# An attention stage and two gated MLPs in split float32 on one core: the norm's sum over partitions as two split products, output tiles stored one by one, and a third weight piece prepared earlier

## The chip, the cores and the metric

The kernel runs on one core of a Trainium2 chip. The metric is the device time of one execution in microseconds. The engines of the core are called PE (TensorE), DVE (VectorE), ACT (ScalarE), POOL (GpSimd) and SP (SyncE, which here only issues transfers).

## What is computed

The reference takes q, k and v of shape (4, 8, 576, 64). For each head it adds two attentions: one over tokens averaged in groups of four, and one over the neighbours closer than four positions. The result, seen as 2304 tokens by 512 features, goes through two MLPs:

```python
h = x @ w_in                                   # 512 -> 2048
x = (max(h, 0) + alpha * min(h, 0)) @ w_out    # 2048 -> 512

xn = x / sqrt(mean(x * x, axis=-1) + 1e-6) * rms_g
g, val = xn @ w_gate, xn @ w_val               # 512 -> 1536, twice
out = (g * sigmoid(g) * val) @ w_out2          # 1536 -> 512
```

## The kernel before

**Split products.** The large products keep float32 accuracy with operands of the type float32r. An operand is written as hi, its rounded copy (made by ACT with a Copy), and lo, the rest (operand minus hi, made by DVE, or by POOL for part of the weights). A product is then three: hi with hi, hi with lo and lo with hi, all summed in one PSUM bank. The weights come in pieces of 128x512; `piece_hi` on ACT and `piece_lo` on DVE or POOL split them. Pieces 0, 2 and 4 (`EARLY`) get their lo from DVE; pieces 6, 8 and 10 (`EARLY_POOL`) are split by POOL alone. The piece 2c is the w_in part that chunk c of the first MLP needs.

**Opening.** The first half batch of attention is computed alone, in an order written out by hand for each engine: `FIRST_PE`, `FIRST_ACT` and `FIRST_DVE`. A letter is a step and the number after it is a head pair: A loads and transposes q and k, B makes scores, P, E and F are the softmax, C transposes the probabilities, D makes the attention's result in `xbuf`. X splits one quarter of the token block (`xhi` by ACT, then `xlo` by DVE), H splits off a weight piece's hi on ACT, L its lo on DVE, and W on PE is work that only keeps the engine busy. Every engine runs its own list in order and waits on semaphores for the others. An H or an X on ACT must precede the L or the X of the same number on DVE; X also needs D of that number done by DVE.

**First MLP.** It goes over 8 blocks of 288 tokens (`TB1`), each in 16 chunks (`C1`) of 128 hidden features. Chunk c: `up` (12 products of 288 columns), then ACT and DVE make the leaky ReLU and its split (`pos`, `neg`, `g1hi`, `g1lo`), and `down` for the chunk two back (12 products). The steps of the next half batch's attention are placed between chunks. In the first block, `up` of chunk 1 waits for the lo of piece 2.

**Second MLP.** It goes over 6 blocks of 384 tokens (`TB2`), each in 12 chunks (`C2`): `up2` is 24 products of 384 columns, `down2` of the chunk two back is 9 products of 512 columns, three for each output tile `y_b[0]`, `y_b[1]`, `y_b[2]` of 128 tokens. The next block's norm is made meanwhile: ACT squares the block (`sq`), DVE sums the four quarters (`ss`, 128x384), PE sums over partitions with a product of a matrix of ones and `ss`, both plain float32, into `ms_b`; ACT takes the root (`norm_root`), and DVE the reciprocal and the scaling (`norm_scale`). The constants say after which chunk ACT and DVE square and sum, when PE multiplies, and when the root and scaling stand in the queues: `NORM1` in the last block of the first MLP (for block 0), `NORM2` in the second MLP:

```python
    NORM1, NORM2 = (5, 10, 10), (6, 7, 7)
```

**Output.** After a block's last `down2`, ACT copies tiles 0 and 2 and DVE copies tile 1 from PSUM to `ysb`. Both wait for `s_g2_used`, which PE raises once after the last product of `down2`; SP stores the tiles in the order 0, 1, 2.

Of the kernel before, what the change touches and what calls it, by code (L numbers as in the profile page):

```python
# [5 lines left out]
def attention_into_two_mlps_kernel(nc: bass.Bass, q, k, v, w_in, w_leaky, alpha, w_gate, w_val, w_out, rms_g, out):  # L6
# [7 lines left out]
    f32, f32r = mybir.dt.float32, mybir.dt.float32r  # L14
# [65 lines left out]
    FIRST_PE = "W8 A0 W2 A1 W2 B0 W2 A2 W3 B1 A3 W6 B2 K0 W1 C0 W1 B3 W4 D0 W8 C1 W3 C2 D1 W1 C3 D2 D3"  # L80
    FIRST_ACT = "A0 A1 A2 P0 E0 A3 P1 E1 C0 H0 P2 E2 D0 P3 E3 C1 X0 K0 C2 D1 C3 D2 X1 D3 X2 X3 H2 H4"
    FIRST_DVE = "A0 A1 B0 A2 B1 F0 A3 B2 B3 F1 D0 F2 F3 X0 D1 L0 D2 X1 D3 X2 X3 L2 L4"

# [16 lines left out]

    NORM1, NORM2 = (5, 10, 10), (6, 7, 7)

# [6 lines left out]
    with ctx:  # L109
# [9 lines left out]
        eps_out = sb("eps_out", [P, 1])  # L119
        ones = sb("ones", [P, P])  # L120
        loaded = ExitStack()
        W_raw = sb("W_raw", [P, Q1, 2, PIECE], f32, loaded)
# [52 lines left out]
        sq = sb("sq", [P, KT * TB2], f32, part2)  # L175
        ss = sb("ss", [P, TB2], f32, part2)
        rinv = sb("rinv", [P, TB2], f32, part2)
        xnhi = sb("xnhi", [P, KT, TB2], f32r, part2)
# [67 lines left out]
        s_sq = sem("s_sq")  # L246
        s_ss = sem("s_ss")
        s_ms = sem("s_ms")
        s_rms = sem("s_rms")
# [8 lines left out]
        s_g2lo = sem("s_g2lo")  # L258
        s_g2_used = sem("s_g2_used")
        s_y_act = sem("s_y_act")  # L260
        s_y_dve = sem("s_y_dve")
# [378 lines left out]
        def _(act):  # L640
# [93 lines left out]
            def norm(i):  # L734
                act.wait_ge(s_x2_in, 16 * i + 16)
                act.activation(sq[:, :], xn[:, :], ACT.Square).then_inc(s_sq, 1)

            def norm_root(i):
                act.wait_ge(s_ms, i + 1)
                act.activation(rinv[:, :], ms_b[:, 0:TB2], ACT.Sqrt, bias=eps6[:, :], scale=1.0 / DM  # L740
                               ).then_inc(s_rms, 1)
# [18 lines left out]
            def y_out(i):  # L760
                act.wait_ge(s_g2_used, C2 * (i + 1) + BEGUN)
                act.wait_ge(s_y_out, 16 * YT * i + BEGUN)
                for t in (0, 2):
                    act.activation(ysb[:, t, :], y_b[t][:, :], ACT.Copy).then_inc(s_y_act, 1)

            def first_mlp(b, half, group, last=False, pieces=False):
                for c in range(C1):
                    run_steps(group, 2 * c)
                    chunk_relu(b, half, c)
                    run_steps(group, 2 * c + 1)  # L770
                    chunk_hi(b, half, c)
                    if pieces:
                        for n in SPLIT_IN_CHUNK[c]:
                            piece_hi(n)
                    if last:
                        for n in LAST_PIECES[c]:
                            piece_hi(n)
                        if c == NORM1[0]:
                            norm(0)
                        if c == NORM1[2]:  # L780
                            norm_root(0)
# [17 lines left out]
            for kind, p, j in first_order(FIRST_ACT):  # L799
# [6 lines left out]
                elif kind in "PE":  # L806
                    first_softmax(kind, p)
                else:
                    attention(0, 0, kind, p, j)
            first_mlp(0, 0, (0, 1), pieces=True)  # L810
            with act.Fori(0, B - 2) as b:
# [6 lines left out]
            def second_mlp(i, more):  # L818
                for c in range(C2):
# [4 lines left out]
                    if more and c == NORM2[0]:  # L824
                        norm(i + 1)
                    if more and c == NORM2[2]:
                        norm_root(i + 1)
# [11 lines left out]
        def _(dve):  # L839
# [123 lines left out]
            def norm(i):  # L963
                dve.wait_ge(s_sq, i + 1)
                dve.tensor_reduce(ss[:, :], sq[:, :].rearrange("p (t s) -> p s t", t=KT), axis=AX.X, op=ALU.add
                                  ).then_inc(s_ss, 1)

            def norm_scale(i):
# [23 lines left out]
            def y_out(i):  # L992
                dve.wait_ge(s_g2_used, C2 * (i + 1) + BEGUN)
                dve.wait_ge(s_y_out, 16 * YT * i + BEGUN)
                dve.tensor_copy(ysb[:, 1, :], y_b[1][:, :]).then_inc(s_y_dve, 1)

            def first_mlp(b, half, group, last=False):
                for c in range(C1):
# [4 lines left out]
                    if last:  # L1003
# [3 lines left out]
                        if c == NORM1[0]:  # L1007
                            norm(0)
                        if c == NORM1[2]:
                            norm_scale(0)  # L1010
# [29 lines left out]
            def second_mlp(i, more):  # L1040
                for c in range(C2):
# [5 lines left out]
                    if more and c == NORM2[0]:  # L1047
                        norm(i + 1)
                    if more and c == NORM2[2]:
                        norm_scale(i + 1)  # L1050
# [11 lines left out]
        def _(pe):  # L1062
# [99 lines left out]
            def norm(i):  # L1162
# [3 lines left out]
                else:  # L1166
                    pe.wait_ge(s_rms, i)
                pe.wait_ge(s_ss, i + 1)
                pe.matmul(ms_b[:, 0:TB2], ones[:, :], ss[:, :], start=True, stop=True).then_inc(s_ms, 1)

            def first_mlp(b, half, group, last=False):
                for c in range(C1):
# [3 lines left out]
                    if c >= LAG1:  # L1176
                        down(b, half, c - LAG1)
                    if last and c == NORM1[1]:
                        norm(0)
# [53 lines left out]
            def down2(i, c):  # L1233
# [7 lines left out]
                for t in range(YT):  # L1241
                    hi, lo = (g[:, c % 3, t * P:(t + 1) * P] for g in (g2hi, g2lo))
                    for j, (g, w) in enumerate(((hi, 0), (hi, 1), (lo, 0))):
                        last = pe.matmul(y_b[t][:, :], g, wpiece(piece, w), start=(c == 0 and j == 0),  # L1244
                                         stop=(c == C2 - 1 and j == 2))
                last.then_inc(s_g2_used, 1)

            def second_mlp(i, more):
                for c in range(C2):
                    up2(i, c)  # L1250
                    if c >= LAG2:
                        down2(i, c - LAG2)
                    if more and c == NORM2[1]:
                        norm(i + 1)
# [33 lines left out]
```

## Time and profile before

| | |
|---|---|
| median of three runs | 1013.38 us (1012.98 to 1015.3) |
| the profiled execution's own time | 1013.07 us |
| its span, first to last instruction | 1011.3 us |
| what lies around the span | 1.8 us |
| mean granted TensorE clock | 0.997 |
| PE busy | 988.5 us, 98% of the span |
| DVE, ACT, POOL busy | 523.4, 403.4, 113.4 us |

A row of the timeline has a start, a duration, the engine, the line, the operation, what it writes and reads, and the count of instructions merged in it; in square brackets stands the idle time of the engine before it and what ended it. Instructions of one engine overlap a little in such rows, so the distance between starts can be shorter than a duration. A matmul's duration contains its way through the array: the distance from one to the next is what a product costs in a stream. The chain of work gives such distances.

### The profile page before, as it was taken

Reading aid. Unit: us, or ns where it says so; the run is one execution under the profiler, and the core shown is the slowest. Engines: PE = TensorE matmul, PEld = TensorE weight load, DVE = VectorE, ACT = ScalarE, POOL = GpSimd, SP = SyncE. Lnnn points to the kernel's source line nnn. Section 1 sums busy time; section 2 is a strip of 40 time slices with the busy share of each in tenths; the row PEclk is TensorE's granted clock in tenths of the full one; section 3 lists DMA queues with packets and bytes.
Section 4 is the critical chain, followed back from the end, with each engine's and each line's share of the span. In section 5 each row is a group of like instructions: output and inputs, shape, how many; then the busy total and the mean of one; then the engine's idle time right before and its main releaser. Section 6 shows DMA issues by size and latency. Waiting matters only on the chain.

```text
span 1011.3 us, 19296 instructions
## 1 busy us (share of the span) xinstructions
PE 988.5 (98%) x7207; PEld 939.7 (93%) x7207; DVE 523.4 (52%) x955; ACT 403.4 (40%) x953; POOL 113.4 (11%) x122
## 2 busy tenths in 40 slices
PE   8889999999999999999999999999999999999998
PEld 7789999998999999999999999999999999999997
DVE  6887875765766757666456453242242242242211
ACT  6656444445444445444455443232232232232211
POOL 3665310002200012000011221000000000000000
PEclk9999999999999999999999999999999999999999
DMA  8931311113201032010154400100100100100000
GB/s 165 267 94 37 95 37 36 33 43 82 51 20 48 11 99 59 20 49 2 52 178 149 121 1 24 40 1 23 40 0 24 38 0 27 36 0 29 4 1 31
DMA packets 98800, 52.19 MB, mean 52 GB/s; under 512 B 60564, under 2 KB 92840, under 8 KB 98728
## 3 DMA queue, kind: packets, MB, share of 16 engines
q1 hardware_dynamic: 94584, 50.14, 17.9%
q10 hardware_dynamic: 4144, 1.03, 0.7%
q8 instruction: 51, 0.84, 0.3%
q14 instruction: 21, 0.17, 0.0%
HBM read 41.72 MB, written 9.44 MB: 51 GB/s over the span
## 4 chain that ended last, share of the span: by engine, by line
PE 90%; DVE 5%; issue 2%; ACT 2%; DMA 1%; SPq 0%; ACTq 0%; DVEq 0%
PE banks L1229 30%; PE banks L1158 19%; PE banks L1144 17%; PE banks L1244 15%; PE banks L1098 2%; PE banks L1125 2%; PE banks L1109 2%; PE banks L1087 1%; DVE pos L945 1%; PE banks L1113 1%; PE banks L1130 1%; PE banks L1101 1%; PE banks L1192 1%; DMA q_tok_first<-in_q_dram 1%; DVE sm L901 0%
## 5 line engine op out<-in xcount | busy, mean ns | idle before, releaser
L1229 PE MATMUL banks<-xnhi,W_front 128*128 128x384 f32 x672 | 175.9, 335 | 0.0
L986 DVE TENSOR_TENSOR g<-banks,silu 128x384 f32<-128x384 f32 x72 | 40.1, 557 | 236.6 <-ACT silu L755 236.6
L1158 PE MATMUL banks<-g1hi,W_front 128*128 128x288 f32 x640 | 145.9, 304 | 0.0
L1144 PE MATMUL banks<-xhi,W_front 128*128 128x288 f32 x640 | 144.5, 302 | 1.2 <-DVE W_front L843 1.0
L755 ACT ACTIVATE silu<-banks 128x384 f32<-128x384 f32 x72 | 35.4, 492 | 259.7 <-PE banks L1229 259.7
L1229 PEld LDWEIGHTS banks<-xnhi,W_front 128*128 128x128 f32 x672 | 121.9, 188 | 1.3
L945 DVE SCALAR_TENSOR_TENSOR pos<-neg,coef,pos 128x288 f32<-128x288 f32 x128 | 76.8, 600 | 81.6 <-ACT neg L718 81.5
L1229 PE MATMUL banks<-xnlo,W_front 128*128 128x384 f32 x336 | 112.4, 335 | 0.0
L1158 PEld LDWEIGHTS banks<-g1hi,W_front 128*128 128x128 f32 x640 | 107.7, 189 | 3.6 <-issue 3.6
L1144 PEld LDWEIGHTS banks<-xhi,W_front 128*128 128x128 f32 x640 | 107.5, 189 | 3.1 <-DVE W_front L843 1.3
L717 ACT ACTIVATE pos<-banks 128x288 f32<-128x288 f32 x128 | 52.2, 408 | 130.5 <-PE banks L1144 130.3
L1229 PE MATMUL banks<-xnhi,W_back 128*128 128x384 f32 x384 | 103.2, 339 | 0.0
L1144 PE MATMUL banks<-xlo,W_front 128*128 128x288 f32 x320 | 94.9, 297 | 0.0
L1158 PE MATMUL banks<-g1lo,W_front 128*128 128x288 f32 x320 | 94.9, 297 | 0.0
L724 ACT ACTIVATE g1hi<-pos 128x288 fp32r<-128x288 f32 x128 | 56.5, 441 | 89.1 <-DVE pos L945 88.7
L952 DVE TENSOR_TENSOR g1lo<-pos,g1hi 128x288 fp32r<-128x288 f32 x128 | 59.0, 461 | 53.5 <-ACT g1hi L724 53.5
L1144 PE MATMUL banks<-xhi,W_back 128*128 128x288 f32 x384 | 84.5, 296 | 0.0
L1158 PE MATMUL banks<-g1hi,W_back 128*128 128x288 f32 x384 | 83.8, 301 | 0.8 <-DVE g1lo L952 0.8
L1229 PEld LDWEIGHTS banks<-xnhi,W_back 128*128 128x128 f32 x384 | 69.7, 188 | 1.5
L1244 PE MATMUL banks<-W_front,g2hi 128*128 128x512 f32 x216 | 67.2, 392 | 0.0
L1158 PEld LDWEIGHTS banks<-g1hi,W_back 128*128 128x128 f32 x384 | 63.3, 188 | 2.3 <-issue 1.2
L1144 PEld LDWEIGHTS banks<-xhi,W_back 128*128 128x128 f32 x384 | 64.2, 188 | 0.1
(151 smaller groups left out, 1894.0 us busy)
## 6 DMA issues: line engine op xcount, KB each, us to landing
W_raw<-in_moe_w_out_dram SPq DMA_DIRECT2D x26, 256.0 KB, 4.8
x_scratch<-xbuf SPq DMA_DIRECT2D x8, 576.0 KB, 3.5
xn<-x_scratch SPq DMA_DIRECT2D x6, 768.0 KB, 4.6
out_dram<-ysb SPq DMA_DIRECT2D x18, 256.0 KB, 2.2
vwin<-in_v_dram SPq DMA_DIRECT2D x90, 51.0 KB
W_raw<-in_moe_w_in_dram SPq DMA_DIRECT2D x16, 256.0 KB, 5.6
q_tok<-in_q_dram SPq DMA_DIRECT2D x56, 72.0 KB, 2.1
v<-in_v_dram SPq DMA_DIRECT2D x26, 144.0 KB
```

Of the source, the lines that this page charges most:

```text
L717: act.activation(pos[:, c % 2, :], hb[c % 2][:, 0:TB1], ACT.Relu).then_inc(s_pos, 1)
L724: act.activation(g1hi[:, c % 3, :], pos[:, c % 2, :], ACT.Copy).then_inc(s_ghi, 1)
L755: act.activation(silu[:, c % 2, :], gate_b[c % 2][:, 0:TB2], ACT.Silu).then_inc(s_silu, 1)
L945: dve.scalar_tensor_tensor(out=pos[:, c % 2, :], in0=neg[:, c % 2, :], scalar=coef[:, c:c + 1], in1=pos[:, c % 2, :], op0=ALU.mult, op1=AL ...
L952: dve.tensor_tensor(g1lo[:, c % 3, :], pos[:, c % 2, :], g1hi[:, c % 3, :].bitcast(f32), ALU.subtract).then_inc(s_glo, 1)
L986: dve.tensor_tensor(g2[:, c % 2, :], val_b[c % 2][:, 0:TB2], silu[:, c % 2, :], ALU.mult).then_inc(s_g2, 1)
L1098: pe.matmul(scores[0:QW, e, w * KW:(w + 1) * KW], qT[rows[e], p % 2, q0:q0 + QW], kT[rows[e], p, k0:k0 + KW], start=True, stop=True)
L1109: pe.transpose(turned[0:KW, e, w * QW:(w + 1) * QW], sm[:, e, w * KW:(w + 1) * KW], ident[0:QW, 0:QW])
L1144: last = pe.matmul(hb[c % 2][:, 0:TB1], w, x[:, t, :], start=(t + j == 0), stop=(t == KT - 1 and j == 2))
L1158: last = pe.matmul(acc[t][:, 0:TB1], w, g[:, c % 3, :], start=(c == 0 and j == 0), stop=(c == C1 - 1 and j == 2))
L1229: last = pe.matmul(bank[:, 0:TB2], w, x[:, t, :], start=(t + j == 0), stop=(t == KT - 1 and j == 2))
L1244: last = pe.matmul(y_b[t][:, :], g, wpiece(piece, w), start=(c == 0 and j == 0), stop=(c == C2 - 1 and j == 2))
```

## The change

Four edits:

1. **Norm.** `ss` is split as other operands are: ACT writes `sshi` (a Copy, 128x384) and DVE writes `sslo` (a subtraction). PE's one float32 product becomes two float32r products, a copy `ones_r` of the ones with `sshi` and with `sslo`, summed in `ms_b`. ACT makes `ones_r` once (128x128), ahead of its first chunk.
2. **Places of the norm.** The constants now mean: square and sum; split; product, root and scaling. `NORM1` is (5, 8, 10): PE's product stays behind chunk 10, the splits come behind chunk 8. `NORM2` is (6, 7, 8): the splits come behind chunk 7, and product, root and scaling move from chunk 7 to chunk 8.
3. **Output tiles.** PE raises a new semaphore `s_y_tile` after the last product of tile 0 and of tile 1. ACT's copy of tile 0 and DVE's copy of tile 1 wait for it; the copy of tile 2 still waits for `s_g2_used`.
4. **Opening.** H2 goes from the end of ACT's list to behind C2. On DVE, L0 goes ahead of D1, L2 from the end to behind D1, and X1 goes ahead of D2.

```diff
-    FIRST_ACT = "A0 A1 A2 P0 E0 A3 P1 E1 C0 H0 P2 E2 D0 P3 E3 C1 X0 K0 C2 D1 C3 D2 X1 D3 X2 X3 H2 H4"
-    FIRST_DVE = "A0 A1 B0 A2 B1 F0 A3 B2 B3 F1 D0 F2 F3 X0 D1 L0 D2 X1 D3 X2 X3 L2 L4"
+    FIRST_ACT = "A0 A1 A2 P0 E0 A3 P1 E1 C0 H0 P2 E2 D0 P3 E3 C1 X0 K0 C2 H2 D1 C3 D2 X1 D3 X2 X3 H4"
+    FIRST_DVE = "A0 A1 B0 A2 B1 F0 A3 B2 B3 F1 D0 F2 F3 X0 L0 D1 L2 X1 D2 D3 X2 X3 L4"
-    NORM1, NORM2 = (5, 10, 10), (6, 7, 7)
+    NORM1, NORM2 = (5, 8, 10), (6, 7, 8)
...
+            def norm_hi(i):
+                act.wait_ge(s_ss, i + 1)
+                if not isinstance(i, int) or i > 0:
+                    act.wait_ge(s_ms, i)
+                act.activation(sshi[:, :], ss[:, :], ACT.Copy).then_inc(s_sshi, 1)
...
             def y_out(i):
-                act.wait_ge(s_g2_used, C2 * (i + 1) + BEGUN)
                 act.wait_ge(s_y_out, 16 * YT * i + BEGUN)
                 for t in (0, 2):
+                    if t == YT - 1:
+                        act.wait_ge(s_g2_used, C2 * (i + 1) + BEGUN)
+                    else:
+                        act.wait_ge(s_y_tile, (YT - 1) * i + t + 1)
                     act.activation(ysb[:, t, :], y_b[t][:, :], ACT.Copy).then_inc(s_y_act, 1)
...
+            act.wait_ge(s_consts, 2 + NW)
+            act.activation(ones_r[:, :], ones[:, :], ACT.Copy).then_inc(s_eps, 1)
             first_mlp(0, 0, (0, 1), pieces=True)
...
+            def norm_lo(i):
+                dve.wait_ge(s_sshi, i + 1)
+                if not isinstance(i, int) or i > 0:
+                    dve.wait_ge(s_ms, i)
+                dve.tensor_tensor(sslo[:, :], ss[:, :], sshi[:, :].bitcast(f32), ALU.subtract).then_inc(s_sslo, 1)
...
             def y_out(i):
-                dve.wait_ge(s_g2_used, C2 * (i + 1) + BEGUN)
+                dve.wait_ge(s_y_tile, (YT - 1) * i + 2)
...
-                pe.wait_ge(s_ss, i + 1)
-                pe.matmul(ms_b[:, 0:TB2], ones[:, :], ss[:, :], start=True, stop=True).then_inc(s_ms, 1)
+                pe.wait_ge(s_eps, 3)
+                pe.wait_ge(s_sslo, i + 1)
+                pe.matmul(ms_b[:, 0:TB2], ones_r[:, :], sshi[:, :], start=True, stop=False)
+                pe.matmul(ms_b[:, 0:TB2], ones_r[:, :], sslo[:, :], start=False, stop=True).then_inc(s_ms, 1)
...
-                    if last and c == NORM1[1]:
+                    if last and c == NORM1[2]:
                         norm(0)
...
+                    if c == C2 - 1 and t < YT - 1:
+                        last.then_inc(s_y_tile, 1)
                 last.then_inc(s_g2_used, 1)
...
-                    if more and c == NORM2[1]:
+                    if more and c == NORM2[2]:
                         norm(i + 1)
```

## Rows read from the trace of the kernel before

**Rows 1.** The page: busy time by engine, and the chain by line.
```profile
PE 988.5 (98%) x7207; PEld 939.7 (93%) x7207; DVE 523.4 (52%) x955; ACT 403.4 (40%) x953; POOL 113.4 (11%) x122
...
PE banks L1229 30%; PE banks L1158 19%; PE banks L1144 17%; PE banks L1244 15%; PE banks L1098 2%; PE banks L1125 2%; PE banks L1109 2%; PE banks L1087 1%; DVE pos L945 1%; PE banks L1113 1%; PE banks L1130 1%; PE banks L1101 1%; PE banks L1192 1%; DMA q_tok_first<-in_q_dram 1%; DVE sm L901 0%
```

**Rows 2.** PE's waits from 34 us on, the largest: total, times, longest.
```profile
PE banks L1109 <- DVE sm L905: 5.0, 5, 1.8
```

**Rows 3.** The chain around a norm product: start, distance, what.
```profile
599.19 0.65 PE banks L1169 x2
599.84 4.17 PE banks L1229 x24
```

**Rows 4.** Timelines of ACT and DVE, one late block of the second MLP.
```profile
901.03 0.53 ACT L758 ACTIVATE g2hi<-g 128x384 fp32r<-128x384 f32 x1 [0.62 <-DVE g L986]
```
```profile
901.59 0.56 DVE L989 TENSOR_TENSOR g2lo<-g,g2hi 128x384 fp32r<-128x384 f32 x1 [0.59 <-ACT g2hi L758]
```

**Rows 5.** Timelines of PE, ACT and DVE in the first MLP's last block.
```profile
541.66 0.37 PE L1158 MATMUL banks<-g1hi,W_back 128*128 128x288 f32 x1 [0.79 <-DVE g1lo L952]
```
```profile
530.71 0.41 ACT L717 ACTIVATE pos<-banks 128x288 f32<-128x288 f32 x1 [0.21 <-PE banks L1144]
...
533.41 1.28 ACT L740 ACT_TABLE_LOAD   x1
```
```profile
530.53 0.69 DVE L843 TENSOR_TENSOR W_front<-W_raw,W_front 128x512 fp32r<-128x512 f32 x1
...
535.32 2.55 DVE L970 RECIPROCAL rinv<-rinv 128x384 f32<-128x384 f32 x1 [1.96 <-ACT rinv L740]
```

**Rows 6.** Timeline of DVE, 30 to 39 us.
```profile
30.75 0.46 DVE L927 TENSOR_TENSOR xbuf<-banks,od 128x288 f32<-128x288 f32 x1
31.12 1.12 DVE L843 TENSOR_TENSOR W_front<-W_raw,W_front 128x512 fp32r<-128x512 f32 x1
32.88 0.46 DVE L927 TENSOR_TENSOR xbuf<-banks,od 128x288 f32<-128x288 f32 x1 [0.63 <-ACT od L701]
...
34.40 2.23 DVE L934 TENSOR_TENSOR xlo<-xbuf,xhi 128x288 fp32r<-128x288 f32 x2
36.56 2.36 DVE L843 TENSOR_TENSOR W_front<-W_raw,W_front 128x512 fp32r<-128x512 f32 x2
```

**Rows 7.** Timelines of POOL, ACT and PE, 30 to 39 us.
```profile
31.10 0.61 POOL L600 CAST W_front<-W_raw 128x512 fp32r<-128x512 f32 x1 [0.35 <-DMA W_raw<-in_moe_w_in_dram]
...
34.25 1.28 POOL L604 TENSOR_TENSOR W_front<-W_raw,W_front 128x512 fp32r<-128x512 f32 x1
...
36.40 1.37 POOL L604 TENSOR_TENSOR W_front<-W_raw,W_front 128x512 fp32r<-128x512 f32 x1
```
```profile
31.71 0.89 ACT L696 ACTIVATE pT<-banks 102x864 f32<-102x864 f32 x1 [0.99 <-PE banks L1113]
```
```profile
34.58 0.44 PE L1087 MATMUL banks<-ident,q_tok 96*128 96x96 f32 x3 [0.92 <-DVE xbuf L927]
...
38.37 0.41 PE L1144 MATMUL banks<-xhi,W_front 128*128 128x288 f32 x1 [1.02 <-DVE W_front L843]
```

**Rows 8.** The end: the chain's last pieces, the stores, SP's wait.
```profile
1000.64 6.18 PE banks L1244 x27
```
```profile
1006.84 1.09 ACT L764 ACTIVATE ysb<-banks 128x512 f32<-128x512 f32 x2 [4.52 <-PE banks L1244]
...
1007.47 1.31 SPq L479 DMA_DIRECT2D out_dram<-ysb  x3
```
```profile
DMA to landing us min/median/max: 2.0/2.4/2.5
```

**Rows 9.** Windows: us, busy PE, PEld, DVE, ACT, POOL, granted clock, DMA share, GB/s.
```profile
67.00:69.00 2.00, 0.48 (x4) 0.24 (x2) 2.00 (x5) 1.19 (x3) 0.15 (x1) 1.00 0.00 0
70.50:75.00 4.50, 4.50 (x26) 4.48 (x25) 3.02 (x5) 3.42 (x7) 3.11 (x3) 0.62 0.15 36
1008.30:1010.40 2.10, 0.00 (x0) 0.00 (x0) 0.00 (x0) 0.00 (x0) 0.00 (x0) 0.79 0.96 373
```

More of the change, by code:

```diff
@@ L120, in attention_into_two_mlps_kernel @@
         ones = sb("ones", [P, P])
+        ones_r = sb("ones_r", [P, P], f32r)
         loaded = ExitStack()
@@ L176, in attention_into_two_mlps_kernel @@
         ss = sb("ss", [P, TB2], f32, part2)
+        sshi = sb("sshi", [P, TB2], f32r, part2)
+        sslo = sb("sslo", [P, TB2], f32r, part2)
         rinv = sb("rinv", [P, TB2], f32, part2)
@@ L247, in attention_into_two_mlps_kernel @@
         s_ss = sem("s_ss")
+        s_sshi = sem("s_sshi")
+        s_sslo = sem("s_sslo")
         s_ms = sem("s_ms")
@@ L259, in attention_into_two_mlps_kernel @@
         s_g2_used = sem("s_g2_used")
+        s_y_tile = sem("s_y_tile")
         s_y_act = sem("s_y_act")
@@ L779, in first_mlp @@
                             norm(0)
+                        if c == NORM1[1]:
+                            norm_hi(0)
                         if c == NORM1[2]:
@@ L825, in second_mlp @@
                         norm(i + 1)
+                    if more and c == NORM2[1]:
+                        norm_hi(i + 1)
                     if more and c == NORM2[2]:
@@ L964, in norm @@
                 dve.wait_ge(s_sq, i + 1)
+                if not isinstance(i, int) or i > 0:
+                    dve.wait_ge(s_sslo, i)
                 dve.tensor_reduce(ss[:, :], sq[:, :].rearrange("p (t s) -> p s t", t=KT), axis=AX.X, op=ALU.add
                                   ).then_inc(s_ss, 1)
+            def norm_lo(i):
+                dve.wait_ge(s_sshi, i + 1)
+                if not isinstance(i, int) or i > 0:
+                    dve.wait_ge(s_ms, i)
+                dve.tensor_tensor(sslo[:, :], ss[:, :], sshi[:, :].bitcast(f32), ALU.subtract).then_inc(s_sslo, 1)
             def norm_scale(i):
@@ L1008, in first_mlp @@
                             norm(0)
+                        if c == NORM1[1]:
+                            norm_lo(0)
                         if c == NORM1[2]:
@@ L1048, in second_mlp @@
                         norm(i + 1)
+                    if more and c == NORM2[1]:
+                        norm_lo(i + 1)
                     if more and c == NORM2[2]:
```

## The prediction

> **What bounds the kernel now.** I read the page first: PE is busy for 98% of the span, and 90% of the chain that ended last runs through its products, while DVE and ACT are busy about half of the time [rows 1]. So an edit counts if it takes work from PE, shortens one of PE's few waits, or shortens what follows PE's last product. The list of PE's waits says where the few are: from 34 us on the largest, 5.0 us in five waits, is for DVE's part of the softmax [rows 2]; one more, of 1.02 us, ends with the lo of a weight piece at 38.37 us [rows 7]. The chain in order of time shows the second MLP without holes: 24 products, 9 products, 24 products, with the norm's product between [rows 3]. So there a shorter product on PE shortens the kernel by its whole difference. At the end PE is done at 1006.82 us (1000.64 + 6.18), and 4.5 us of copies and stores follow up to the span's end at 1011.3 [rows 8].
>
> **The norm's products.** The chain has 0.65 us for one norm product, recorded as two instructions [rows 3]. The split form is two products of 384 columns from SBUF, like those of `up2`: 24 of these take 4.17 us, so one takes 0.174 and two take 0.35 us [rows 3]. The saving is 0.30 us each time, six times. The ones are already loaded as weights before each of the two instructions; nothing is added there.
>
> What is added lies on ACT (`sshi`, 128x384, as the `g2hi` copy: 0.53 us) and DVE (`sslo`, as the `g2lo` subtraction: 0.56 us) [rows 4]. In the second MLP both are hidden. Counted in that timeline, the copy follows `g2hi` of chunk 7 (ends 901.56) and ends at 902.1, the subtraction at 902.7. PE now wants it one chunk later than it took `ss`, and a chunk is 4.17 + 6.18/3 = 6.2 us [rows 3, 8]. PE's next work after 901.6 is that of chunk 8, so its product stands near 908, 5 us after `sslo`. Behind the subtraction on DVE waits `g` of chunk 8, due with PE's next `up2`, some 4 us later. In block 0 the weight pieces stand ahead of `sshi`, at most three copies; the 5 us hold them.
>
> The root, reciprocal (2.55 us [rows 5]) and four scalings move one chunk back. They hold up `g` of chunk 9 instead of 8, whose `g2lo` PE wants only in the `down2` two chunks later, 12 us on; `split_xn` comes after chunk 11 and still finds them done. I cost the move at nothing. Without its cover it would cost up to 2 us per block.
>
> The first of the six is different. In the last block of the first MLP PE waits 0.79 us at 541.66 for a `g1lo` that stands behind DVE's reciprocal and scalings [rows 5]. The reciprocal started at 535.32 behind ACT's root, and the root behind a table load begun at 533.41, which waited for ACT's own queue and not for PE's product [rows 5]. A product shorter by 0.30 us makes only PE's wait longer by 0.30. And ACT now has `sshi` (0.53 us) to do in chunk 8, ahead of which the only spare time I find is the 0.21 us before `pos` at 530.71 [rows 5]: 0.3 us passes on to root, reciprocal and PE. So the norm gives 5 x 0.30 - 0.3 = 1.2 us. Bounds: 1.8 (all six count, no delay) and 0.9 (the 0.53 passes on whole and the subtraction's 0.56 costs a little more).
>
> **The opening.** H2 (0.6 us) fits on ACT: it starts when C2's copy ends, about 30.5, and ACT is idle for 0.99 us up to 31.71 [rows 7]. Piece 2 was requested at 18 us; its transfer is not late. On DVE, L2 leaves the tail of the list and goes into a stretch with 0.63 us of idle before 32.88 [rows 6]. But the rows show that DVE's subtractions do not run freely beside POOL. Alone the subtraction of a weight piece takes 0.69 us [rows 5]; L0 at 31.12, begun just behind POOL's cast, took 1.12, and L2 with L4, begun at 36.56 when POOL was in its own subtraction until 37.77, took 2.36 for both [rows 6, 7]. X2, begun at 34.40 inside POOL's 34.25 to 35.53, came so late that X2 and X3 took 2.23 [rows 6, 7]. So whichever began second finished after the first. I replay the order with that:
>
> - L0 runs at about 30.6 to 31.3, before POOL's cast; D1 follows to 31.8; L2 waits for the cast and ends near 32.4. POOL is pushed back by 0.2 us.
> - X1, which now stands ahead of D2, waits for POOL's first subtraction: 33.9. D2 and D3 follow to 34.7 instead of 34.5. PE's A step starts at 34.8, not 34.58.
> - X2 and X3 come between POOL's pieces as before, 0.2 later; POOL ends at 38.0 instead of 37.77. Only L4 is left: it ends near 38.4, where L2 and L4 ended at 38.92.
> - PE's chunk 1 no longer waits for L2: it starts behind chunk 0, near 37.55, not 38.37.
>
> PE is 0.8 us ahead, DVE's queue 0.5. PE's next long waits are for DVE [rows 2], so 0.5 is what stays. Bounds: a gain of 1.0 (the whole wait) if DVE and POOL don't hold each other up, a loss of 0.2 if L2 pushes POOL back by its full length and L4 comes behind that. The nearest rows are those of L2 and L4, so I take 0.5. `ones_r` (a small copy, as a weight piece's quarter) lies before the first chunk, where ACT waits for PE anyway, and the ones and masks are ready at 31 us, before POOL's cast starts.
>
> On why L0 and L2 stretch: the Trainium skill, page "SBUF — State Buffer", section "Who interferes with whom", says that a DVE instruction with two inputs in SBUF and a GpSimd instruction that reads SBUF take the shared read port in turn, each whole. The trace agrees as far as these rows go. By the rule the opening gives the 0.5; taken as free of each other, the two engines would give 1.0 and the sum would be 0.5 lower.
>
> **The end.** Now tile 0 is ready on PE two thirds of a `down2` before the end (1006.82 - 1.37 = 1005.45), tile 1 at 1006.14. After 1006.82 one copy of 0.6 us remains instead of ACT's two (1.09 us [rows 8]). Today the stores are issued from 1007.47 on, 0.44 us each, so the third at 1008.34 [rows 8]. After: the third at 1007.47, 0.87 earlier. It also finds the queue empty: today three stores of 256 KB run together from 1008.3 to 1010.4 at 373 GB/s [rows 9], about 0.7 us each, and the third lands latest. With the first two gone ahead, it should land in the shortest time, 2.0 us, not in 2.5 [rows 8]. That is up to 1.35 us; 0.9 is the lower end (issue alone). I take 1.2. Inside the loop the earlier copies change nothing, as PE's next use of these banks is three `up2` away.
>
> **Sum.** 1.2 + 0.5 + 1.2 = 2.9 us. Against the profiled execution: 1013.07 - 2.9 = 1010.2. The median is 0.3 above that execution; I forecast 1010.3. The difference that a measurement of this kernel can tell from none is about 0.2%, 2.0 us, so this is faster by 0.29%.
>
> **Rivals.**
> *The opening gives nothing back* (chance 0.25). POOL and DVE hold each other up so that L4 ends no earlier; PE's chunk 1 starts early and the gain is lost at PE's next softmax wait. With the norm at 0.9 and the end at 0.9 to 1.2: 1.6 to 2.1 us, about 1011.4. For it: three subtractions and two casts of POOL lie in the same 6.7 us as six of DVE's. Against it: DVE has idle time there now.
> *All parts give their full value* (0.15): 1.5 + 1.0 + 1.35 = 3.9 us, 1009.3. It needs DVE and POOL to interleave better than today.
> *The clock falls more often* (0.08), the rival on the other side. At 70.5 to 75 us the granted clock was 0.62 on average, after PE had been busy only 0.48 of 2.00 us at 67 to 69 [rows 9]. That is one stretch at the lower level (1.2 instead of 2.4 GHz), and costs 4.5 x 0.38 = 1.7 us. The change moves PE's waits in the opening by about a microsecond; a second fall would give 1012.0, and from two more falls on the kernel is slower than before: 1013.7. Against it: the change shortens waits there, and adds none. If the fall vanishes instead, 1008.6.
> The Trainium skill, page "TensorE: Matmul & The Clock Gate", section "What's actually happening", says that low activity takes the clock down and that the moment shifts from run to run. The trace shows one fall after idle time; how it shifts no single trace can show.
> *The split doesn't shorten the product* would leave 0.5 + 1.2 - 0.3 = 1.4 us, 1011.8; the 24 products in 4.17 us speak against it, and I count it with the first rival.
>
> **How the numbers follow.** The forecast has 0.52. Its own range, from its bounds, is 1009.4 to 1011.2. With the cases beside it, 8 times in 10 the time should lie in 1008.7 to 1012.0. Faster by over 0.2% is the forecast but its upper edge, the full value, and a little of the first rival: 0.68. Within 0.2%: most of the first rival, one more fall of the clock: 0.28. Slower: 0.04.
>
> **What would show it.** The chain should have 0.35 us for a norm product; PE should go from `up2` to `down2` without any wait for `sslo`; the wait at 541.66 should grow from 0.79 to about 1.4. The wait for the piece at 38.37 should be gone, and DVE's L4 should end near 38.4. After PE's last product 3.2 to 3.6 us should follow, not 4.5. The prediction is wrong if `sslo` holds PE up, if L4 ends at 39 or later, or if the granted clock has more or fewer falls than one.

## The result, and the profile after

| | before | after |
|---|---|---|
| median of 13 runs each | 1013.38 us (1012.26 to 1016.06) | 1011.58 us (1010.22 to 1015.0) |
| ratio of the times, 95% interval | | 0.9975 [0.9964, 0.9987] |
| the profiled execution's own time | 1013.07 us | 1010.22 us |
| its span | 1011.3 us | 1008.4 us |
| its mean granted TensorE clock | 0.997 | 1.000 |

The change makes the kernel faster by 0.25%, 2.5 us (0.0025 x 1013.38), within 1.3 and 3.6. The two medians lie 1.8 us apart, which is within that interval too. The median is 1.3 us above the forecast of 1010.3. It is inside the wide range (1008.7 to 1012.0) and 0.4 us outside the forecast's own (1009.4 to 1011.2), close to the rival in which the opening gives nothing back (1011.4). The profiled pair differs by 2.85 us, where the sum said 2.9; that the two agree so well is luck, as the account of the opening below shows.

The page of the kernel after, busy time by engine and the chain by line:

```profile
PE 985.5 (98%) x7207; PEld 938.1 (93%) x7207; DVE 528.8 (52%) x961; ACT 406.4 (40%) x960; POOL 114.7 (11%) x122
...
PE banks L1266 30%; PE banks L1193 17%; PE banks L1179 16%; PE banks L1281 15%; DVE pos L968 2%; PE banks L1133 2%; PE banks L1160 2%; PE banks L1144 2%; PE banks L1122 1%; PE banks L1148 1%; PE banks L1165 1%; PE banks L1136 1%; PE banks L1229 1%; DVE sm L924 1%; ACT W_front L658 1%
```

PE is still the bound, busy for 3.0 us less than in [rows 1]. The lines have moved: L1179 is `up`, L1193 `down`, L1266 `up2`, L1281 `down2`.

The chain around a norm product (start, distance, what), which answers to [rows 3]:

```profile
605.21 0.17 PE banks L1205
605.38 0.18 PE banks L1206
605.55 4.18 PE banks L1266 x24
```

The two split products take 0.35 us where one float32 product took 0.65. They follow `down2` without a wait, and no wait of PE for `sslo` is in the trace.

The first MLP's last block, timelines of PE, ACT and DVE (start, duration, what, idle time before it), which answer to [rows 5]:

```profile
541.42 0.37 PE L1193 MATMUL banks<-g1hi,W_back 128*128 128x288 f32 x1 [0.92 <-DVE g1lo L975]
```
```profile
527.64 0.51 ACT L750 ACTIVATE sshi<-ss 128x384 fp32r<-128x384 f32 x1
...
529.98 0.45 ACT L732 ACTIVATE g1hi<-pos 128x288 fp32r<-128x288 f32 x1 [1.24 <-DVE pos L968]
...
533.18 1.28 ACT L754 ACT_TABLE_LOAD   x1
```
```profile
528.18 1.34 DVE L997 TENSOR_TENSOR sslo<-ss,sshi 128x384 fp32r<-128x384 f32 x1 [0.48 <-ACT sshi L750]
...
535.09 2.55 DVE L1001 RECIPROCAL rinv<-rinv 128x384 f32<-128x384 f32 x1 [1.96 <-ACT rinv L754]
```

PE's wait is 0.92 us where 1.4 was forecast (0.79 before). The table load, which the forecast pushed back by 0.3 us, begins 0.23 earlier than before, at the same distance from PE's wait (8.24 us; 8.25 before): the added copy did not reach it.

The opening, timelines of DVE and PE, which answer to [rows 6, 7]:

```profile
29.88 0.45 DVE L877 TENSOR_TENSOR sm<-sm,rsum 96x288 f32<-96x288 f32 x1
...
30.69 0.75 DVE L866 TENSOR_TENSOR W_front<-W_raw,W_front 128x512 fp32r<-128x512 f32 x1
...
31.73 0.67 DVE L866 TENSOR_TENSOR W_front<-W_raw,W_front 128x512 fp32r<-128x512 f32 x1
...
35.78 1.78 DVE L866 TENSOR_TENSOR W_front<-W_raw,W_front 128x512 fp32r<-128x512 f32 x1
37.49 0.44 DVE L914 TENSOR_REDUCE qd<-qT 128x72 f32<-128x288 f32 x1
```
```profile
34.47 0.44 PE L1122 MATMUL banks<-ident,q_tok 96*128 96x96 f32 x3 [1.05 <-DVE xbuf L950]
54.30 0.46 PE L1144 MATMUL banks<-ident,sm 96*102 96x96 f32 x3 [1.72 <-DVE sm L928]
```

The wait for piece 2 is gone, as forecast, and L4 ends at 37.56. But the softmax wait near 55 us is longer, 1.72 us for 1.45: PE arrives earlier and gives a part back. DVE's L0 and L2 take 0.75 and 0.67 us here. Both are done before POOL's first cast of a piece, which stands at 32.72 us, behind the masks, where it stood at 31.10 before [rows 7]. What took longer beside them are POOL's masks: 2.34 us for three of them, for 1.70 before.

```profile
30.42 2.34 POOL L600 TENSOR_SCALAR_AFFINE_SELECT mask<-mask 96x102 f32<-96x102 f32 x3
32.72 0.60 POOL L608 CAST W_front<-W_raw 128x512 fp32r<-128x512 f32 x1
```

The end: the chain's last pieces, then the copies and the stores on their engines, which answer to [rows 8]:

```profile
998.99 6.18 PE banks L1281 x27
1005.17 0.02 issue
1005.19 0.60 ACT ysb L781
```
```profile
1003.89 0.60 ACT L781 ACTIVATE ysb<-banks 128x512 f32<-128x512 f32 x1 [3.22 <-PE banks L1281]
...
1004.51 0.69 DVE L1026 COPY ysb<-banks 128x512 f32<-128x512 f32 x1 [3.25 <-PE banks L1281]
1004.51 1.63 SPq L487 DMA_DIRECT2D out_dram<-ysb  x3
...
1005.19 0.60 ACT L781 ACTIVATE ysb<-banks 128x512 f32<-128x512 f32 x1 [0.70 <-PE banks L1281]
```

PE ends at 1005.17 and the span at 1008.4: 3.2 us follow, where 4.5 followed before. The first two copies lie beside `down2`.

### The profile page after: what moved, and what is told of

Same layout as the page of the kernel before. It is cut to its first block, busy times and chain, and to the rows that moved or that the text cites. A ratio compares the mean times of both kernels' runs of the same rounds, so it can differ in the third digit from the quotient of the medians.

```text
span 1008.4 us, 19333 instructions
## 1 busy us (share of the span) xinstructions
PE 985.5 (98%) x7207; PEld 938.1 (93%) x7207; DVE 528.8 (52%) x961; ACT 406.4 (40%) x960; POOL 114.7 (11%) x122
## 4 chain that ended last, share of the span: by engine, by line
PE 87%; DVE 6%; issue 3%; ACT 3%; DMA 1%; SPq 0%; DVEq 0%; ACTq 0%
PE banks L1266 30%; PE banks L1193 17%; PE banks L1179 16%; PE banks L1281 15%; DVE pos L968 2%; PE banks L1133 2%; PE banks L1160 2%; PE banks L1144 2%; PE banks L1122 1%; PE banks L1148 1%; PE banks L1165 1%; PE banks L1136 1%; PE banks L1229 1%; DVE sm L924 1%; ACT W_front L658 1%
## 5 line engine op out<-in xcount | busy, mean ns | idle before, releaser
L1266 PE MATMUL banks<-xnhi,W_front 128*128 128x384 f32 x672 | 176.0, 335 | 0.0
L1193 PE MATMUL banks<-g1hi,W_front 128*128 128x288 f32 x640 | 145.5, 303 | 0.0
L1179 PE MATMUL banks<-xhi,W_front 128*128 128x288 f32 x640 | 143.2, 301 | 0.0
L1266 PEld LDWEIGHTS banks<-xnhi,W_front 128*128 128x128 f32 x672 | 121.9, 188 | 1.3
L1266 PE MATMUL banks<-xnlo,W_front 128*128 128x384 f32 x336 | 112.5, 335 | 0.0
L1193 PEld LDWEIGHTS banks<-g1hi,W_front 128*128 128x128 f32 x640 | 107.2, 188 | 4.0 <-issue 3.8
L1179 PEld LDWEIGHTS banks<-xhi,W_front 128*128 128x128 f32 x640 | 106.8, 188 | 1.2 <-issue 1.2
L1266 PE MATMUL banks<-xnhi,W_back 128*128 128x384 f32 x384 | 101.8, 335 | 0.0
L1179 PE MATMUL banks<-xlo,W_front 128*128 128x288 f32 x320 | 94.7, 296 | 0.0
L1193 PE MATMUL banks<-g1lo,W_front 128*128 128x288 f32 x320 | 94.6, 296 | 0.0
L1193 PE MATMUL banks<-g1hi,W_back 128*128 128x288 f32 x384 | 83.7, 301 | 0.9 <-DVE g1lo L975 0.9
L1179 PE MATMUL banks<-xhi,W_back 128*128 128x288 f32 x384 | 84.3, 296 | 0.0
L1266 PEld LDWEIGHTS banks<-xnhi,W_back 128*128 128x128 f32 x384 | 69.8, 188 | 0.9
L1281 PE MATMUL banks<-W_front,g2hi 128*128 128x512 f32 x216 | 67.2, 392 | 0.0
L1193 PEld LDWEIGHTS banks<-g1hi,W_back 128*128 128x128 f32 x384 | 63.3, 188 | 2.4 <-issue 1.3
L1266 PE MATMUL banks<-xnlo,W_back 128*128 128x384 f32 x192 | 64.3, 335 | 0.0
```

The costliest lines, as they stand in the source:

```text
L1179: last = pe.matmul(hb[c % 2][:, 0:TB1], w, x[:, t, :], start=(t + j == 0), stop=(t == KT - 1 and j == 2))
L1193: last = pe.matmul(acc[t][:, 0:TB1], w, g[:, c % 3, :], start=(c == 0 and j == 0), stop=(c == C1 - 1 and j == 2))
L1266: last = pe.matmul(bank[:, 0:TB2], w, x[:, t, :], start=(t + j == 0), stop=(t == KT - 1 and j == 2))
```

## The experiments

The ratios are against the kernel before on the same chip, whose medians were 1013.40 us (35 runs), 1013.53 (25) and 1013.47 (29) for the three groups of experiments. "Changed" is the kernel after.

**One part at a time.** The opening alone, twice:

```diff
 (kernel before)
-    FIRST_ACT = "... C2 D1 C3 D2 X1 D3 X2 X3 H2 H4"
-    FIRST_DVE = "... X0 D1 L0 D2 X1 D3 X2 X3 L2 L4"
+    FIRST_ACT = "... C2 H2 D1 C3 D2 X1 D3 X2 X3 H4"
+    FIRST_DVE = "... X0 L0 D1 L2 X1 D2 D3 X2 X3 L4"
```

> The kernel before with the two lists of the opening alone changed (H2, L0, L2 and X1 moved). Theory 1, the opening's gain lasts: in the changed kernel PE's softmax step that had waited at 55.44 us starts at 54.30, 1.14 us earlier, so the whole time should be about 1.1 us lower (ratio 0.9989) and the first norm product of the second MLP's preparation, at 532.1 us before, should start near 531.0. Theory 2, the opening gives nothing in the end: the same 1.1 us at 54 us, but it is eaten by PE's waits for DVE in the first MLP's loops before 541 us, as in the changed kernel, where the lead at 541.66 was only 0.24 us: ratio 0.9998 or above, the wait for g1lo near 541.5. Theory 3, the lead in the opening comes from POOL starting its pieces at 32.7 instead of 31.1 us in that one execution: then this run, with POOL at 31.1, has L4's end near 38.4 and a lead of 0.5.

> The opening alone once more, since its 0.5 us is small against the spread of runs. The fit over all runs so far, with the mean granted clock as a second variable, gives it +0.04 us with an error of 0.22. Theory 1 (0.5 us gained) would give 0.9995; theory 2 (nothing) 1.0000; the first measurement was 1.0011 [0.9999, 1.0023]. A second value above 1.0005 would speak for a loss.

Measured: 1014.48 us, 1.0011 [0.9999, 1.0023], and 1014.19 us, 1.0011 [0.9995, 1.0026], 12 runs each. The opening alone brings nothing that can be measured. In the first run's timelines of DVE and POOL:

```profile
30.55 1.53 DVE L843 TENSOR_TENSOR W_front<-W_raw,W_front 128x512 fp32r<-128x512 f32 x1
...
32.38 1.64 DVE L843 TENSOR_TENSOR W_front<-W_raw,W_front 128x512 fp32r<-128x512 f32 x1
```
```profile
31.62 1.84 POOL L604 TENSOR_TENSOR W_front<-W_raw,W_front 128x512 fp32r<-128x512 f32 x1
```

L0 and L2 take 1.53 and 1.64 us beside POOL, for 0.75 and 0.67 in the profile after. L4 ends at 39.27 (39.02 in the second run), not near 38.4; but the clock is down in both profiles, so they don't settle where it ends at full clock. And there are falls of the clock just there. Windows of this run (us, busy PE, PEld, DVE, ACT, POOL, granted clock, DMA share, GB/s):

```profile
34.00:38.00 4.00, 2.77 (x31) 2.59 (x28) 2.85 (x5) 2.24 (x7) 3.82 (x4) 0.50 0.76 234
38.00:42.00 4.00, 4.00 (x22) 4.00 (x22) 2.14 (x5) 0.92 (x3) 0.00 (x0) 0.66 0.91 258
```

A granted clock of 0.50 is the lower level, 1.2 GHz.

The norm alone (splits, two products and places as in the change), and the tiles alone:

```diff
 (norm alone: the kernel changed, with the opening's lists and this as before)
-                    if t == YT - 1:
-                        act.wait_ge(s_g2_used, C2 * (i + 1) + BEGUN)
-                    else:
-                        act.wait_ge(s_y_tile, (YT - 1) * i + t + 1)
+                act.wait_ge(s_g2_used, C2 * (i + 1) + BEGUN)
...
-                dve.wait_ge(s_y_tile, (YT - 1) * i + 2)
+                dve.wait_ge(s_g2_used, C2 * (i + 1) + BEGUN)
```

> The kernel before with the split norm product and its places alone; the opening and the output tiles as before. My reckoning: five times 0.30 us gained, the first of the six loses 0.3, together 1.2 us (ratio 0.9988). Rival: the first of the six neither gains nor loses, 1.5 us (0.9985), with the wait at 541.66 us at 0.9 to 1.1 instead of 1.4. Rival on the other side: moving root, reciprocal and scaling one chunk back costs waits in the second MLP, seen as PE idle there; then less than 1 us. Between the first and the last norm product of the trace the distance shrinks by 1.5 us in any case, less such waits.

```diff
 (tiles alone: the kernel before, with)
+                    if c == C2 - 1 and t < YT - 1:
+                        last.then_inc(s_y_tile, 1)
...
+                        act.wait_ge(s_y_tile, (YT - 1) * i + t + 1)
...
+                dve.wait_ge(s_y_tile, (YT - 1) * i + 2)
```

> The kernel before with the output tiles leaving one by one alone. My reckoning: what follows PE's last product shrinks from 4.5 to 3.3 us, and the time by 1.2 us (ratio 0.9988). Rival: the stores of tiles 0 and 1 take descriptors or bandwidth from the last one, so that only 0.9 us is gained. Nothing before PE's last product should differ.

Measured: norm alone 1011.66 us, 0.9990 [0.9975, 1.0004]; tiles alone 1012.83 us, 0.9993 [0.9980, 1.0007]. Each interval still holds no change; the traces are sharper. From the `down` at which PE waits for `g1lo` (541.66 before) to the end of PE's last product it is 465.16 us before and 465.17 with the tiles alone, but 463.75 to 463.78 in the profiles of the change, of its repetition, of the norm alone, and of norm and tiles together. So the norm saves 1.4 us behind that point. The two profiles of the opening alone have 465.17 as well, and the later profile with POOL held back has 463.75: all with the one float32 product agree, and all with the split one. With the tiles alone, the chain's end is

```profile
1000.88 6.18 PE banks L1248 x27
1007.06 0.02 issue
1007.08 0.60 ACT ysb L768
```

and the span 1010.2: 3.1 us after PE, for 4.5.

**The change once more, and without its opening.** In the second kernel the two lists are those of before.

> The changed kernel once more, word for word, to see how far two executions of the same program differ in their traces. If the sum of the parts holds, 2.9 us less than before (ratio 0.9971); by the 13 runs so far 2.5 us (0.9975). If the lead of the opening is lost always at the same place, PE's waits for DVE stand where they stood in the first trace (one of 0.50 us near 389 us). If it is chance, they stand elsewhere.

> The changed kernel with the two lists of the opening put back as they were before: norm and output tiles only. Theory 2 (the opening gives nothing in the end; the opening alone was 1.0011 [0.9999, 1.0023]): this is as fast as the whole change, 2.4 to 3.0 us below the kernel before, ratio 0.9970 to 0.9976. Theory 1 (the opening's 0.5 to 1.1 us last): this is 0.5 to 1.1 us slower than the whole change, ratio 0.9980 or above.

Measured: the change 1010.51 us, 0.9967 [0.9953, 0.9980]; norm and tiles without the opening 1010.67 us (7 runs), 0.9972 [0.9961, 0.9983]. Leaving the opening out costs nothing that shows. As to the places of PE's waits for DVE's softmax: the repetition has the wait near 389 us again (0.57 us, at 391.54), but so do kernels with the old lists (0.50 at 390.88 with norm, tiles and scalings apart), so it doesn't come from the opening's edit. The one of 0.71 at 257.33 is not in the repetition, which has 0.72 at 140.57 instead.

**Only the places of the norm's product and root.** The kernel before, with product, root and scaling behind chunk 8:

```diff
-    NORM1, NORM2 = (5, 10, 10), (6, 7, 7)
+    NORM1, NORM2 = (5, 10, 10), (6, 8, 8)
```

> The kernel before with nothing but the product, root, reciprocal and scaling of the second MLP's norm moved from chunk 7 to chunk 8. My reckoning: no effect, ratio 1.0000, PE without a wait in the second MLP. Rival: the norm part gained more than 1.2 us because the new place helps; then this is 0.3 to 0.7 us faster by itself. If the place costs, up to 2 us per block slower.

Measured: 1014.43 us, 1.0013 [0.9999, 1.0027]. The chain still goes through the second MLP without a hole, with the long product in its new place:

```profile
610.00 0.65 PE banks L1169 x2
610.64 4.17 PE banks L1229 x24
```

From the `down` near 541 to the end of PE's last product it is 465.16 us here too. So the later place costs nothing on PE and gives nothing; the shorter product gives the norm's gain.

**POOL held back in the opening.** The kernel changed; POOL starts its pieces only when DVE has done L2:

```diff
                 if n in EARLY_POOL:
+                    pool.wait_ge(s_wlo[0], 2)
                     wait_piece(pool, n)
```

> The changed kernel, with POOL's work on the weight pieces 6, 8 and 10 held back until DVE has done L2. If DVE's weight subtractions stretch because POOL's casts and subtractions hold what both need, L0 and L2 take 0.67 to 0.75 us each here, in every execution, where in the opening beside POOL they took 1.53 and 1.64 (the opening alone). POOL's three pieces then end some 2 us later and collide with X2, X3 and L4 and with piece 1 instead, so the whole time should not fall: level with the changed kernel or up to 1 us slower. Rival: L0 and L2 stretch for another reason, and take over 1 us here too.

Measured: 1011.38 us (10 runs), 0.9978 [0.9967, 0.9990]. DVE's timeline:

```profile
31.64 0.75 DVE L867 TENSOR_TENSOR W_front<-W_raw,W_front 128x512 fp32r<-128x512 f32 x1
...
32.75 0.68 DVE L867 TENSOR_TENSOR W_front<-W_raw,W_front 128x512 fp32r<-128x512 f32 x1
34.39 1.45 DVE L958 TENSOR_TENSOR xlo<-xbuf,xhi 128x288 fp32r<-128x288 f32 x1 [0.96 <-ACT xhi L715]
```

With POOL held back L0 and L2 take 0.75 and 0.68 us (one profile); what they gain, X1 loses (1.45 us, for 0.67 in the profile after), because it now meets POOL. The time isn't measurably better than the change's.

**The wait that is left in the first MLP.** DVE's reciprocal and four scalings stand in one piece ahead of a `g1lo`. Here the scalings of block 0 come two chunks behind the reciprocal; in the last kernel one scaling in each of the chunks 11 to 14:

```diff
-                        if c == NORM1[2]:
-                            norm_scale(0)
+                        if c == NORM1[2]:
+                            norm_recip(0)
+                        if c == NORM1[2] + 2:
+                            norm_mul(0)
```

With the change's opening:

> The changed kernel, with DVE's four scalings of block 0 put two chunks behind its reciprocal in the last block of the first MLP (chunk 12 instead of 10). If PE's wait of 0.92 us near 541.4 us comes from reciprocal and scalings standing together ahead of g1lo, it disappears, and the time falls by a further 0.9 us against the changed kernel. Rival: the wait only moves two chunks back, and the time stays.

With the opening of before, twice:

> Norm and output tiles with the opening as before, and block 0's scalings two chunks behind the reciprocal. If both readings hold (the opening is worth nothing, the wait of 0.92 us goes away) this is the fastest or level with the changed kernel with scalings apart: about 3.5 us below the kernel before, ratio 0.9965. If the opening is worth its 0.5 us, it is 0.5 us behind that one.

> The fastest so far once more (0.9956 [0.9943, 0.9969] from 5 runs), to see if it holds: by the fit over all runs so far norm -1.4, end -1.0, scalings apart -0.5 us, together -2.9 us, ratio 0.9971; by the first measurement 0.9956.

And with the opening of before, one scaling for each chunk:

```diff
+                        if 1 <= c - NORM1[2] <= KT:
+                            norm_mul(0, (c - NORM1[2] - 1,))
```

> As the last one, with the four scalings of block 0 put one behind each of the chunks 11 to 14. With all four behind chunk 12 PE still waited 0.74 us for g1lo near 551 us; one scaling of 0.6 us in a chunk of 3.3 us fits into DVE's idle time, so no such wait should be left between 535 and 560 us, and the time should be 0.7 us lower than with the scalings at chunk 12. Rival: the reciprocal alone (2.55 us) holds g1lo up, and a wait stays.

Measured: 1010.48 us, 0.9968 [0.9953, 0.9983]; 1008.97 us (5 runs), 0.9956 [0.9943, 0.9969]; 1010.73 us, 0.9973 [0.9955, 0.9991]; spread 1009.73 us (6 runs), 0.9967 [0.9955, 0.9980]. PE's wait in the first of them, and in the spread kernel:

```profile
551.17 0.37 PE L1198 MATMUL banks<-g1hi,W_back 128*128 128x288 f32 x1 [0.74 <-DVE g1lo L975]
```
```profile
550.38 0.37 PE L1198 MATMUL banks<-g1hi,W_back 128*128 128x288 f32 x1 [0.35 <-DVE g1lo L975]
```

Moving the scalings in one piece moves the wait with them (0.92 at 541 becomes 0.74 at 551); spreading them leaves 0.35. That is 0.6 us off PE's path. None of these intervals lies clear of the change's own, so no best version is shown; norm, tiles and spread scalings without the opening's edit have the shortest span of all profiles, 1007.5 us.

**All runs together.** Every run has its time and its mean granted clock. The 213 runs of the experiments, 89 of them of the kernel before, fitted by least squares with a term for each part and one for the clock (95% is about twice the figure behind the sign; what is left has a standard deviation of 1.0 us):

```
kernel before at full clock   1012.52 +- 0.12 us
opening                         +0.09 +- 0.17
norm                            -1.47 +- 0.24
tiles                           -1.08 +- 0.24
places alone                    +0.12 +- 0.31
POOL held back                  -0.57 +- 0.39
scalings two chunks later       -0.40 +- 0.28
scalings spread                 -1.47 +- 0.46
each 0.001 of mean clock lost   +0.51 +- 0.02
```

The parts sum to 2.5 us, as the ratio of the first comparison says. The 13 runs of the kernel after from that comparison are not among the 213; with them norm and tiles come out at -1.39 and -1.00, the opening at +0.16, the sum at 2.2 us. The last line is why the single kernels' intervals are wide: the clock of a run goes down to 0.990, which is 5 us, more than the whole change. The spread kernel's 1.5 us rests on 6 runs and is more than the 0.6 that its trace shows; I trust the trace.

## Why the prediction held, step by step

**The norm: 1.2 forecast, 1.4 measured.** Five products in the second MLP give 5 x 0.28 = 1.4 us on PE's path, and `sshi`, `sslo` and the later root stay hidden, as worked out. What failed is the term for the loss in the first MLP's last block, 0.3 us. I let the added ACT copy pass through to the table load. It ran at 527.64, one chunk earlier than the `pos` at whose 0.21 us of idle time I looked, and ACT then waits 1.24 us for DVE's `pos` before the next `g1hi` (the row at 529.98 above); the copy disappears in that wait.

DVE's `sslo` took 1.34 us there (0.55 elsewhere). It pushed `g1hi` back by 0.5 us (529.98, 3.21 behind the `g1hi` ahead of it; before 529.53, 2.68 behind), and one chunk later nothing of that is left (532.20, where it was 532.43): ACT's wait for `pos` there is 0.65 us instead of 1.01, and the 0.21 us of idle time is gone. PE's wait grew by 0.13 us, less than the 0.30 by which its product became shorter. The norm is 1.4 to 1.5 us by trace and fit, within the bounds of 0.9 to 1.8.

**The tiles: 1.2 forecast, 1.25 measured** (4.48 us after PE's last product, then 3.23), and 1.08 +- 0.24 by the fit. The stores land in 2.1 to 2.2 us each, for 2.0, 2.4 and 2.5 before: most of it is the earlier issue (the last copy ends 0.6 us behind PE), the rest the third store, which runs with less beside it. That the queue is emptier is my reading of these times; no experiment varied it.

**The opening: 0.5 forecast, 0.34 and 0.64 near 55 us in two traces, none that the runs can show.** This is the term that was mis-sized. The wait for piece 2 went as forecast, and DVE's queue is what counts behind it, as argued. To see its size I take a mark ahead of the edit, the last piece of DVE's step F3 (`sm<-sm,rsum 96x288`, start at 29.88 in the rows above), and go from there to the ends of PE's waits near 55 and 110 us, in the profiles whose clock is full from that mark up to 60 us:

```
                                   F3 to softmax wait   F3 to the wait near 110
before                                   25.78                81.09
tiles alone                              25.06                80.35
norm and tiles                           25.07                80.29
norm, tiles, scalings apart (again)      25.05                80.30
norm, tiles, scalings spread             25.05                80.25
after                                    24.42                79.67
changed, scalings apart                  24.72                79.94
```

Four kernels with the old lists agree within 0.02 us at the first wait and within 0.10 at the second. Against them the change's lists gain 0.34 us in one kernel, where POOL's first cast starts 0.52 us behind F3 (31.20 and 30.68), as it does in those four (0.51). In the profile after POOL is 2.84 us behind F3, and the gain is 0.64. In the profile of before POOL is 1.44 behind, and it lies 0.72 above the four: how DVE and POOL meet differs from one execution to the next, and there they met badly. I read L0 with 1.12, X2 and X3 with 2.23 from this one execution and took them for the kernel's own; with norm and tiles and the same lists they take 1.72 and 1.53. The opening's part of the profiled pair, 1.36 us (25.78 - 24.42), is therefore for the most part how two executions fell out, and it does not last: at the `down` near 541 the kernel after leads by only 0.24 us (541.66 and 541.42). On the way it has waits of 0.71 us at 257.33 and 0.50 at 388.84 for DVE's softmax, of which the kernel before shows at most 0.16 (it has one of 0.71 at 139.01, where the kernel after has 0.17: the lead was 1.75 us there before it shrank). The distance from 110 to 541 us varies from 430.1 to 432.1 us among all profiles, edited opening or not; what sets it in one execution stays open. So a few tenths gained at 55 us aren't seen in the end: +0.09 +- 0.17. The pair's 2.85 us is then, to the rounding of the spans, 0.24 up to 541, 1.39 in PE's path behind it, and 1.25 behind PE. The forecast's 2.9 is met by a norm and an end that gave a little more than forecast and by a lead up to 541 that is an accident of two executions.

That DVE and POOL hold each other up is shown: L0 takes 0.75 us with POOL away and 1.53 and 1.31 beside it in the two profiles of the opening alone. L2 takes 1.64 in the first of these; in the second it takes 0.67, and POOL's subtraction beside it 2.56 instead of 1.27:

```profile
32.30 0.67 DVE L843 TENSOR_TENSOR W_front<-W_raw,W_front 128x512 fp32r<-128x512 f32 x1
```
```profile
31.54 2.56 POOL L604 TENSOR_TENSOR W_front<-W_raw,W_front 128x512 fp32r<-128x512 f32 x1
```

Here L2 began second and finished first, at 32.97 against 34.10. So the rule by which I replayed the order, that whichever began second finished after the first, does not hold in every execution. The Trainium skill's page "SBUF — State Buffer", section "Who interferes with whom", has a DVE instruction with two SBUF inputs and a GpSimd instruction that reads SBUF take the shared port in turn. The trace of the held-back POOL agrees that the two hold each other up, down to X1, which pays (1.45 us) when it is the next to meet POOL. Turns taken by whole instructions in the order of their starts don't come out of the pair above.

**The clock.** Its rival had 0.08, as something that the change brings. The fall at 70.5 us of the profile before [rows 9] is missing in the profile after, so one of the prediction's own signs of being wrong (more or fewer falls than one) appeared. But the runs don't show that the opening's edit changes how often there are falls: a mean clock below 0.998 in 62 of 155 runs with the old lists and in 29 of 58 with the new, with means of 0.9971 +- 0.0002 and 0.9969 +- 0.0004. The difference of the means is worth 0.1 us, and the fit's term for the opening holds it apart. What was wrong is the idea of one fall to add or lose: falls differ from run to run, mostly between 28 and 44 us.

The price of that fall was wrong too: 4.5 x 0.38 = 1.7 us of lost clock, but only 0.1 us of time. PE's softmax waits near 69 and 83 us end 13.95 us apart before (69.26 and 83.21) and 13.82 after (68.13 and 81.95), and 13.92 with the tiles alone, whose profile has the same fall. Where the clock falls, PE comes later to the second wait, and the wait is shorter. Before, then after:

```profile
83.21 0.46 PE L1109 MATMUL banks<-ident,sm 96*102 96x96 f32 x3 [0.37 <-DVE sm L905]
```
```profile
81.95 0.46 PE L1144 MATMUL banks<-ident,sm 96*102 96x96 f32 x3 [1.80 <-DVE sm L928]
```

So this fall's absence explains at most 0.1 us of the profiled pair. A fall in the opening costs more. The windows of the kernel with only the places moved, the slowest profile (1017.62 us):

```profile
26.00:28.00 2.00, 1.01 (x12) 1.05 (x13) 1.93 (x5) 1.70 (x11) 1.92 (x5) 1.00 0.89 243
28.00:30.00 2.00, 1.38 (x12) 1.22 (x11) 1.93 (x5) 1.31 (x4) 1.73 (x5) 0.68 0.94 263
30.00:32.00 2.00, 2.00 (x23) 1.84 (x23) 1.11 (x3) 0.89 (x1) 1.11 (x2) 0.50 0.85 290
```

PE is busy for 1.0 and 1.4 of 2.0 us and the clock falls to 1.2 GHz; it stays there to about 42 us. From F3 (30.30) to the softmax wait (59.47) this profile takes 29.17 us, 4.1 more than the four above, for some 6 us of lost clock. In the profile before PE was busy for 1.3 and 1.4 us in the same windows and the clock held.

**The chances.** I gave the opening without gain 0.25. The forecast stood on one profile for a term of 0.5 us; the four later profiles with the old lists say that a single reading of such a stretch is uncertain by 0.7. The sum's own range was narrower than its terms: the lower bounds add up to 0.9 - 0.2 + 0.9 = 1.6 us and the upper to 1.8 + 1.0 + 1.35 = 4.15, which is 1009.0 to 1011.6 and not 1009.4 to 1011.2. The measured 1011.58 is at that edge. Two slips of the text changed nothing: in the 6.7 us of the first rival POOL has three casts, not two, and if DVE and POOL were free of each other it is the time that would be 0.5 us lower, not the sum of the gains.

## What to carry to other kernels

Where PE is the bound and its chain has no holes, a plain float32 product in it is worth splitting, even if two other engines must split its operand first: each of five here gave 0.28 us, and the split cost nothing because it lay in waits (the sixth, ahead of a wait for DVE, gave PE mostly a longer wait). Let each output tile go when it is ready; it shortens only the very end, but it shows in every profile: 3.1 to 3.3 us behind PE's last product in the nine with the edit, 4.4 to 4.5 in the five without. Reordering by hand in a stretch where two engines hold each other up should be judged from several profiles, with distances from a mark ahead of the edit: one profile there was off by 0.7 us. And a fall of the clock is not to be priced by its lost clock alone: look at the next wait behind it.

## What the runs showed of the hardware

- A float32 product of 384 columns takes PE 0.65 us in the chain, and two float32r products of the same shape 0.35, one 0.174: a factor of 3.7 for each product.
- A subtraction of 128x512 on DVE takes 0.67 to 0.75 us, and up to 1.72 beside POOL's casts and subtractions; POOL's subtraction itself goes from 1.27 to 1.84 us and once 2.56.
- The kernel before, run 89 times, lies between 1011.64 and 1018.56 us, and most of that is its mean granted clock, from 1.000 down to 0.990: 0.51 us for each 0.001. A loss of 0.001 is 2.0 us of the 1010 at the lower level, 1.0 us of PE's work; half of it is seen in the time. One reason is in the traces: the fall at 70.5 us was taken up by PE's next wait, down to 0.1 us, and one in the opening cost 4.1 us of 6. Whether that accounts for the whole half was not worked out.
